# Own term of the first four units: a feature-wise product summed by PE instead of two row-wise Pool products and a DVE sum

## What is computed

```python
for t in range(S):
    kt, vt, rt, wt = (k[:, :, t], v[:, :, t], r[:, :, t], w[:, :, t])
    cur = np.einsum('bhd,bhe->bhde', u[None] * kt, vt)
    y[:, :, t] = np.einsum('bhd,bhde->bhe', rt, state + cur)
    state = wt[:, :, :, None] * state + np.einsum('bhd,bhe->bhde', kt, vt)
...
h = np.maximum(x @ w_in, 0.0)
return (h * h @ w_out).astype(np.float32)
```

## Time and profile before

| | us |
|---|---|
| median of 3 runs | 779.87 |
| lowest and highest | 778.12, 780.2 |
| the profiled execution's own time | 779.41 |
| its span in the trace | 777.8 |
| PE busy | 755.1 (97%) |
| DVE busy | 469.6 (60%) |
| ACT busy | 323.7 (42%) |
| Pool busy | 229.3 (29%) |

### The profile page before, as it was taken

How to read it: one execution, slowest core, us unless ns; L and a number is a source line. 1 busy time by engine, 2 the same in 40 slices (tenths; PEclk the granted TensorE clock), 3 DMA queues, 4 the chain that set the end, 5 groups by cost and what they waited for, 6 DMA issues and landing times.

```text
span 777.8 us, 15695 instructions
## 1 busy us (share of the span) xinstructions
PE 755.1 (97%) x5571; PEld 661.1 (85%) x5571; DVE 469.6 (60%) x756; ACT 323.7 (42%) x636; POOL 229.3 (29%) x213
## 2 busy tenths in 40 slices
PE   6799999999999999999999999999999999999994
PEld 3488888888988888888888899998999999999994
DVE  8977887866586576676486645334542246353861
ACT  3555544434333334434344323253432255253841
POOL 7834423312242222421042210262431112211211
PEclk9999999999999999999999999999999999999998
DMA  9875222321132223322331005154661126616610
GB/s 231 270 227 186 69 67 86 109 62 41 44 111 63 62 63 102 93 62 62 101 95 40 23 33 203 58 190 138 227 233 61 61 62 214 224 55 224 212 52 7
DMA packets 50195, 87.99 MB, mean 113 GB/s; under 512 B 5932, under 2 KB 33560, under 8 KB 50128
## 3 DMA queue, kind: packets, MB, share of 16 engines
q1 hardware_dynamic: 41376, 61.01, 27.5%
q0 software_dynamic: 7648, 24.51, 8.7%
q10 hardware_dynamic: 1104, 1.57, 0.6%
HBM read 72.78 MB, written 16.75 MB: 115 GB/s over the span
## 4 chain that ended last, share of the span: by engine, by line
PE 91%; DVE 3%; ACT 1%; issue 1%; POOL 1%; DMA 1%; SPq 0%; DVEq 0%; POOLq 0%; ACTq 0%
PE bank L602 27%; PE bank L604 25%; PE bank L603 25%; PE bank L654 3%; PE bank L874 3%; PE bank L683 2%; PE bank L699 2%; PE bank L729 1%; PE bank L663 1%; PE bank L821 1%; ACT spare L978 1%; DVE spare L1215 1%; DVE work L1193 1%; PE bank L688 1%; PE bank L693 1%
## 5 line engine op out<-in xcount | busy, mean ns | idle before, releaser
L602 PE MATMUL bank<-wo_hi,h_hi 128*128 128x394 f32 (+1 forms) x576 | 201.6, 350 | 1.0 <-DVE h_lo L1505 1.0
L604 PE MATMUL bank<-wo_hi,h_lo 128*128 128x394 f32 (+1 forms) x576 | 196.1, 340 | 0.0
L603 PE MATMUL bank<-wo_lo,h_hi 128*128 128x394 f32 (+1 forms) x576 | 195.6, 340 | 0.0
L1383 DVE SCALAR_TENSOR_TENSOR hid<-bank,hid 128x512 f32<-128x512 f32 x96 | 65.2, 679 | 135.0 <-ACT hid L1020 135.0
L1020 ACT ACTIVATE hid<-bank 128x512 f32<-128x512 f32 x96 | 57.0, 594 | 158.3 <-PE bank L604 149.9
L602 PE MATMUL bank<-xt_hi,wi_hi 128*128 128x512 f32 x288 | 116.5, 405 | 0.3 <-DVE xt_lo L1259 0.3
L602 PEld LDWEIGHTS bank<-wo_hi,h_hi 128*128 128x128 f32 x576 | 108.3, 188 | 9.0 <-issue 3.0
L604 PE MATMUL bank<-xt_hi,wi_lo 128*128 128x512 f32 x288 | 113.0, 392 | 0.0
L603 PE MATMUL bank<-xt_lo,wi_hi 128*128 128x512 f32 x288 | 112.7, 391 | 0.0
L603 PEld LDWEIGHTS bank<-wo_lo,h_hi 128*128 128x128 f32 x576 | 108.5, 188 | 2.9
L1604 POOL TENSOR_TENSOR work<-work 112x512 f32<-112x512 f32 x24 | 35.6, 1484 | 251.6 <-DVE work L1193 249.7
(11 more groups left out here) (152 smaller groups left out, 1221.3 us busy)
## 6 DMA issues: line engine op xcount, KB each, us to landing
work<-rkw SPq DMA_DIRECT2D x48, 192.0 KB, 3.8
spare<-rk_rows SPq DMA_DIRECT2D x22, 384.0 KB, 4.2
work<-sorted_rows SPq DMA_DIRECT2D x24, 193.0 KB
work<-rkw SPq DMA_DIRECT2D x48, 96.0 KB, 3.3
work<-v_rows SPq DMA_DIRECT2D x24, 192.0 KB, 3.9
x_cur<-sorted_rows SPq DMA_DIRECT2D x24, 192.0 KB
work<-w POOLq DMA_DIRECT2D x6, 768.0 KB, 7.4
x<-w POOLq DMA_DIRECT2D x6, 768.0 KB, 10.1
```

What stands on the lines that cost most here:

```text
L602: pe.matmul(ps, a_hi, b_hi, start=start, stop=False, skip_group_check=True)
L603: pe.matmul(ps, a_hi, b_lo, start=False, stop=False, skip_group_check=True)
L604: return pe.matmul(ps, a_lo, b_hi, start=False, stop=stop, skip_group_check=True)
L1383: dve.scalar_tensor_tensor(hid[:, f % 2, :], HID[f % 2][:, :], 0.0, hid[:, f % 2, :], ALU.max, ALU.mult).then_inc(sb_sq, 1)
```

## The change

For the four units of chunk 0 the own term takes another way. `first_own` on Pool multiplies r by k as they lie in `rk_in`, features on partitions, before `receptance` and `keys` change them in place. `own_products` on PE takes the result as weights, four pairs, and multiplies it by `u_two`, a tile with u in two columns per pair (one per half, the rest zero), which gives 128x8 in the bank HID[0]. `take_own` on ACT copies that into `own_sum` and raises `own_summed` in DVE's place. Gone for these units are the four loads of `rk_rows`, `own_rows` on Pool and `own_term` on DVE. `own_u` is loaded later, for unit 4. `u_two` comes by two loads of 48x4 single numbers from one row of `u_rows`. `load_mlp_piece(1)` moves up. On PE `own_products` stands behind `head_scores` of the unit before, and in unit 2 `keep_busy(2)` gives way to `keep_busy_rounded`, 12 products of 128x256 in rounded fp32. Units from 4 on are as before.

```diff
+        u_two = sb("u_two", [T, PAIRS, 2])
...
             def load_own(c, b):
                 unit = B * c + b
-                if isinstance(c, int) and 2 <= unit <= B:
-                    sp.wait_ge(own_summed, unit - 1)
-                elif not isinstance(c, int) or unit > 2:
-                    sp.wait_ge(own_summed, unit)
+                sp.wait_ge(own_summed, B - 1 if isinstance(c, int) and unit == B else unit)
...
-            load_own(0, 0)
-            sp.dma_start(own_u[:, :], u_rows).then_inc(u_loaded, 16)
             load_rk(0, 0, 1)
             sp.wait_ge(const_v, 2)
             load_rk(0, 0, 0)
+            for half in range(2):
+                p = slice(HALF * half, HALF * half + D)
+                src = u_rows[0:1, :].rearrange("x (j a d) -> a d (x j)", a=2, d=D)
+                sp.dma_start(u_two[p, :, half], src[half], allow_slow_non_contiguous=True).then_inc(u_two_loaded, 16)
...
-            load_own(0, 1)
...
-            load_own(0, 2)
             load_mlp_piece(0)
             early_decays(3)
             early_rk(2)
             early_v(2)
-            load_own(0, 3)
             load_transposed(0)
+            load_mlp_piece(1)
             early_rk(3)
             early_v(3)
             early_decays(4)
+            sp.dma_start(own_u[:, :], u_rows).then_inc(u_loaded, 16)
             load_own(1, 0)
-            load_mlp_piece(1)
...
-            keep_busy(6)
+            def own_products(b):
+                pe.wait_ge(own_done, 2 * b + 2)
+                if b > 0:
+                    pe.wait_ge(own_summed, b)
+                rows = by_time(own_of(0, b)[:, 0:PAIRS * T])
+                for j in range(PAIRS):
+                    last = pe.matmul(HID[0][:, 2 * j:2 * j + 2], rows[0:PK, j, :], u_two[0:PK, j, :],
+                                     start=(j == 0), stop=(j == PAIRS - 1), skip_group_check=True)
+                last.then_inc(ps_own, 1)
+            def keep_busy_rounded():
+                for _ in range(4):
+                    for k in range(KD):
+                        pe.matmul(HID[1][:, 0:2 * T], xt_hi[0][:, k, 0:T], wi_hi[:, k, 0:2 * T], start=True, stop=True)
+            keep_busy(3)
+            pe.wait_ge(u_two_loaded, 32)
+            own_products(0)
+            keep_busy(2)
             for b in range(B):
                 head_scores(0, b)
-                if b == 1 or b == 2:
+                if b < B - 1:
+                    own_products(b + 1)
+                if b == 1:
                     keep_busy(2)
+                if b == 2:
+                    pe.wait_ge(w_hi, 1)
+                    keep_busy_rounded()
                 k_transpose(0, b)
...
+            def take_own(b):
+                act.wait_ge(ps_own, b + 1)
+                act.activation(own_sum[:, b % 2, :], HID[0][:, 0:H], ACT.Copy).then_inc(own_summed, 1)
...
             keep_decay(0)
+            take_own(0)
             own_diagonal(0, 0)
...
                 if b < B - 1:
+                    take_own(b + 1)
                     own_diagonal(0, b + 1)
...
+            def first_own(b):
+                pool.wait_ge(loaded[b % 2], (b // 2) * 32 + 32)
+                if b > 1:
+                    pool.wait_ge(own_summed, b - 1)
+                pool.tensor_tensor(by_time(own_of(0, b)[:, 0:PAIRS * T])[0:PK], rk_in[b % 2][0:PK, 0],
+                                   rk_in[b % 2][0:PK, 1], ALU.mult).then_inc(own_done, 2)
...
-            for b in range(2):
-                factors(0, b, own_first=True)
-            own_rows(0, 2)
-            receptance(0, 2)
-            keys(0, 2)
-            factors(0, 3, own_first=True)
+            for b in range(B):
+                first_own(b)
+                receptance(0, b)
+                keys(0, b)
             own_rows(1, 0)
```

More of the change, by code:

```diff
@@ L205, in build @@
         u_loaded = sem("u_loaded")
+        u_two_loaded = sem("u_two_loaded")
+        ps_own = sem("ps_own")
         pad_set = sem("pad_set")
@@ L1224, in own_term @@
                 dve.wait_ge(own_done, 2 * unit + 2)
-                if not isinstance(c, int) or unit > 1:
-                    dve.wait_ge(sb_diag, unit - 1)
+                dve.wait_ge(sb_diag, unit - 1)
                 dve.tensor_reduce(own_sum[:, n, :], own_of(c, b)[:, 0:DM].rearrange("p (h d) -> p h d", h=H), AX.X,
@@ L1438, in _ @@
             dve.memset(x_cur[:, 0:KD * GW], 0.0)
+            dve.memset(u_two[:, :, :], 0.0)
             dve.memset(rk_in[0][32:64].rearrange("p a j t -> p (a j t)"), 1.0).then_inc(const_v, 1)
@@ L1454, in _ @@
             inverses(0, 0)
-            own_term(0, 0)
             decays(0, 1)
@@ L1460, in _ @@
             inverse(0, 1, 1)
-            own_term(0, 1)
             for b in range(2):
@@ L1466, in _ @@
                 mask_scores(0, b + 1, 1)
-                own_term(0, b + 2)
                 take_xlo(0, 0, b)
@@ L1609, in own_rows @@
                 n = b % 2
-                pool.wait_ge(own_loaded[n], (2 * c + b // 2) * 16 + 16)
-                if isinstance(c, int) and unit == 0:
+                pool.wait_ge(own_loaded[n], (2 * c + b // 2 - 2) * 16 + 16)
+                if isinstance(c, int) and unit == B:
                     pool.wait_ge(u_loaded, 16)
@@ L1626, in keys, with factors @@
                                    ).then_inc(k_done, 1)
[L1628 to L1635, removed]
+            def factors(c, b):
+                receptance(c, b)
+                own_rows(c, b)
                 keys(c, b)
```

## The result

The changed kernel took **788.42 us** (median of 4 runs, 787.27 to 790.63) against 779.2 of the kernel before (a fourth run, 778.53, has moved its median from 779.87): a ratio of 1.0122, 95% interval 1.0092 to 1.0152. It is 9.2 us slower; 779.0 had been predicted, and even the range ended at 781.0. The profiled execution took 787.27 with a span of 785.7 us, 7.9 more than the 777.8 of before. The profiled execution is the fastest of the four; how the 9.2 us of the medians divide was not traced.

A forecast was written before the change was run, and what follows sets the result against it. The start-up chain to `layer1`'s first product at 40.75 us was taken as the bound; unit 2's new wait left the mask at 34.75, not 35.20, so -0.45 us from 779.41: 779.0 rounded, range 776.9 to 781.0.

The forecast's parts named there:

- Unit 0: Start-up, first unit: Pool and PE finish sooner, scores at 11.7 + 1.16, mask near 13.05, a gain of 0.8 us.
- rival 4: Ahead of unit 0's scores: the two `u_two` loads land late and move the chain by 2.2, giving 781.2; chance 0.10.
- The sums: DVE in units 1 and 2: each dropped sum frees 0.41 us; the scan of 2.18 was left unchanged.
- A new wait in unit 2: PE waits for Pool's product of unit 3; transposition of unit 2 at 30.5, leaving 0.3 of 1.6 us gained.
- Transposition of unit 1: On PE, 23.95 before, to come 0.8 + 0.4 us earlier, at 22.75.
- From there to Pool's product: From unit 1's transposition to Pool's use of r and k of unit 3: 4.53 us, so 27.3.
- Own products: On PE, 4 matmuls with two columns: at most the 0.60 of four transpositions, taken as 0.5 us.
- Rounded fillers: On PE in unit 2, 12 rounded products: at least 1.4 us, 2.3 if weight loads paced them, taken as 1.5.
- rival 1: In unit 3 the clock stays up because the rounded products are denser: 1.3 us more gained, 777.7; chance 0.20.
- rival 3: In unit 2 PE's idle lowers the clock; transposition and attention lose 1.3 us, mask at 36.0, 780.2; chance 0.18.
- nothing else in this change can: Whole kernel: only moving `layer1`'s first product, at 40.75 us, moves the end, and by as much.
- The moved weights: Load queue ahead of r and k of unit 3: 768 KB priced at nothing, up to 2 to 3 us if still in flight.

The follow-up runs named there:

- experiment 1: Changed kernel with three one-column memsets of an unused tile added ahead of DVE's loop; 783.24 us, 1.0053 of before.
- experiment 4: Changed kernel with the next unit's own products put behind the present unit's attention on PE, not ahead of its key transposition; 784.3 us.
- experiment 5: Changed kernel without the fillers of units 1 and 2 (two filling products and twelve rounded ones); 785.38 us.
- experiment 7: Changed kernel with three memsets ahead of DVE's loop and the fillers of units 1 and 2 ahead of the own products; 779.82 us, 1.0009 of before.
- experiment 2: Kernel before the change, with three of DVE's memsets moved to Pool; 784.77 us.
- experiment 9: `load_mlp_piece(1)` put back behind `load_own(1, 0)`, in changed kernel with three memsets: 780.41 us with fillers ahead of own products, 783.34 in the change's own order.
- these last two kernels: Changed kernel with three memsets, fillers first and the weights load put back, 780.41 us; the same with one filler less ahead of unit 0's scores, 779.35.

## Why the prediction was wrong

**What held.** The bound was read rightly: `layer1`'s delay came through to the end one to one (4.03 of 4.0 in experiment 1; in the six other kernels without the stall the two differ by 0.0 to 0.9). Unit 0 gained 1.2 us, 0.8 having been priced (mask at 12.64, 13.05 predicted). The two loads of `u_two`, rival 4, cost nothing: PE came to them at 8.34 without a wait. (The prediction has 9.5; its own rows give 9.1, 12.08 less three fillers of 0.99.) The sums did hold DVE up, even more than priced: the mask of unit 1 is 2.6 us earlier, at 20.02 in place of 22.61, partly by the scan, 1.17 and not 2.18. And Pool's product of unit 3, not DVE, decides unit 2.

**The first failed step: "A new wait in unit 2".** It says "PE then does own products (0.5, to 29.0) and 12 rounded products" and "The transposition of unit 2 comes at 30.5". It came at 35.97. Along the step's own terms:

- Transposition of unit 1: 22.75 predicted, 25.12 measured, +2.4. The same wait stood one unit earlier and was not priced: `own_products(2)` waits for Pool's product of unit 2, whose start at 18.98 is 3.9 us after its load was issued at 15.07. That paragraph counted only DVE.
- From there to Pool's product: 4.53 predicted, 5.09 measured, and 0.13 in the product and behind it: +0.7.
- Own products: 0.5 predicted, 1.72 to the next row, +1.2. They take 0.95 at the full clock and 1.87 at half.
- Rounded fillers: 1.5 predicted, 2.71 to the next row, +1.2. They ran at half clock.

These are the 5.5 us. Another 0.9 came with ACT's diagonal, still partly at half clock (it ends 5.06 behind the transposition, not 4.19), and 1.2 came back, since the last transposition ran at the full clock (4.32 from the last mask to `layer1`, not 5.55): the effect of rival 1, not seen coming together with rival 3. That rival, "The wait costs the clock", comes nearest, but it was priced once, at 1.3 us, for transposition and attention. What stands directly behind the wait are own products and fillers, and they pay first. That the wait for Pool's product is what brought the clock down is not shown: in the change the clock fell just behind it, but in experiment 1 the stretch from 19 to 20 us already has a mean of 0.69, ahead of that wait, and in experiment 4 it fell without one. The bound for the own products, the 0.60 of four transpositions, was too low even at the full clock (0.95). Pool's products of units 2 and 3, for which PE waited, kernel after:

```profile
18.98 1.29 POOL L1654 TENSOR_TENSOR spare<-work 112x512 f32<-112x512 f32 x1 [1.22 <-issue]
...
30.21 1.27 POOL L1654 TENSOR_TENSOR stage<-work 112x512 f32<-112x512 f32 x1 [7.57 <-issue]
```

The profile puts these waits of Pool under "issue", not under the load. That r and k released it is inferred: each of their four loads landed 3.0 to 3.6 us after its issue, and the later one of each pair was issued some 0.4 us behind the first (15.07, 26.11). So the pairs were complete at 18.5 to 19.1 and at 29.5 to 30.1, by this estimate.

Stretch up to 41 us, kernel after:

```profile
0.00:41.00 41.00, 32.40 (x302) 23.28 (x302) 29.21 (x33) 15.68 (x48) 25.43 (x32) 0.79 0.63 173
```

The same stretch before:

```profile
0.00:41.00 41.00, 28.98 (x318) 18.28 (x319) 35.06 (x42) 18.46 (x49) 34.02 (x41) 0.92 0.91 258
```

PE is busy for 3.4 us longer with 16 matmuls less: at a granted clock of 0.79 in place of 0.92 a busier engine does less. That order causes the loss, and not the own products' work, is shown by experiments 4, 5 and 7, each with an edit of its own.

**The second failed step: "and nothing else in this change can".** The change's sums were priced as time that DVE gets back. They are also instructions ahead of its loop. With three fewer the loop's body lies otherwise in DVE's program, and its second pass stalls in "issue" with 3 or 4 packets on q14 in place of 1. Experiments 1 and 2 show it from both sides, and the spans of experiment 1 and the change, 3.9 apart, are 0.7 in `layer1` and 3.2 here. The medians differ by 5.2 and, in experiment 2, by 5.8. Experiment 2's span is 5.3 over before: 3.5 of idle, 0.8 by which its DVE is already late ahead of the gap, and 1.0 left over. In the profiled executions with this stall and a mean clock of 0.91 to 0.96 around it, 0.9 to 2.0 us are left over beyond the wait and the shift of `layer1` (in experiment 2 the 0.8 and the 1.0 together); in that of the change, with 1.00, nothing is. How much of this remainder is the clock's, and how much of it is in the medians, was not measured.

On instruction fetch the Trainium skill, "Runtime: NRT & Kernel Launch", section "Instruction fetch mechanics", says that the sequencer of most engines holds only two blocks of 256 instructions and that a taken branch whose target is not among them must fetch before execution goes on. The idle "issue" and the extra packets agree with that in kind, but that it is the cause is argued: the size of a block no run here shows, and neither the engine that q14 serves nor the instruction that crosses an edge was traced. What the runs show is that the place of the loop in DVE's program decides.

**Priced at nothing.** The moved weights cost nothing in the change's own order (experiment 9, 783.34 against 783.24), as predicted, since there Pool's product came no later with the move (4.4 us behind the transposition of unit 1, 4.9 with the load put back); in the order of experiment 7 they delayed Pool's product by 1.5 us (6.4 against 4.87 behind the transposition). Still open is why the median did not follow: the runs of these last two kernels spread over 4.9 and 9.5 us, those of the kernel before beside them over 4.9, and the last transposition ran at half clock in both profiled executions, which lie below their medians all the same. What the runs above the medians lose no profile shows.

## What to carry to other kernels

Where one engine takes its instructions in order, look at every unit of the loop for the operand that each moved instruction waits for, not only at the unit where the wait is expected; put ready work and fillers ahead of the wait, since behind it they delay what is ready, and here ran at half clock besides (3.4 us from order alone). An edit that changes how many instructions stand ahead of a hardware loop can cost at the jump back, whatever the instructions do: compare that place in the two traces for "issue" idle and packets on the instruction queue, and try the kernel with the count restored before judging the edit.

## What was not expected of the hardware

The stall at the loop's second pass comes and goes with a single instruction: late with 0, 1 and 2 memsets put back (3.3, 3.5 and 3.5 us), gone with 3. Four products with 112x128 weights and only 2 columns (8 instructions) take 0.95 to 1.05 us at the full clock, more than four transpositions of 112 columns (0.58 to 0.60). When a DVE scan and Pool's keys overlapped, the one that started later was stretched, in these rows. In the same unit the keys, begun at 16.93, took 1.27 and the scan, begun at 17.11, took 2.18 before; after, the scan came first, at 15.53, and took 1.17, and the keys, begun at 15.76, took 2.01. So the prediction's price for the keys, 2.20 beside a scan, is borne out only where the keys start second.
